# First maxima by transfers on ACT's queue, dense filler products among the first tiles, first weight slices prepared further ahead

## What is computed

```python
# attention, for each batch and head, t = 0..767
m_new  = maximum(f_gate[t] + m, i_gate[t])
f_stab = exp(f_gate[t] + m - m_new);  i_stab = exp(i_gate[t] - m_new)
C = f_stab * C + i_stab * outer(v[t], k[t])
n = f_stab * n + i_stab * k[t]
y[t] = sigmoid(o_gate[t]) * (C @ q[t]) / maximum(abs(n @ q[t]), 1.0)
...
# x: (3072, 320), w_in: (320, 2048), w_out: (2048, 320)
x = maximum(x @ w_in, 0) ** 2 @ w_out                      # first layer
h = x @ w_in2                                              # second layer
x = where(h > 0, h, exp(minimum(h, 0)) - 1) @ w_out2
```

## Time and profile before

| | us |
|---|---|
| median of 3 runs | 880.08 |
| lowest, highest | 879.46, 881.64 |
| the profiled execution, device time | 878.74 |
| its span, first to last instruction | 877.0 |

### The profile page before, as it was taken

The page is one execution under the profiler, slowest core; times in us unless marked ns, Lnnn a source line. Parts: engine busy times, 40 slices in busy tenths (PEclk is TensorE's granted clock), DMA queues, the critical chain, the costliest instruction groups (busy, mean ns, idle before and its releaser), DMA issues.

```text
span 877.0 us, 15290 instructions
## 1 busy us (share of the span) xinstructions
PE 858.6 (98%) x5633; PEld 838.5 (96%) x5633; DVE 514.6 (59%) x879; ACT 436.7 (50%) x955; POOL 379.0 (43%) x409
## 2 busy tenths in 40 slices
PE   9996899999999999999999999999999999999998
PEld 7876899999999999999999999999999999999998
DVE  4478888777678587775763764444444444444443
ACT  2274566465565565655734654434444443434343
POOL 2155564454444444543532754333334343433333
PEclk9997999999999999999999999999999999999999
DMA  6265443335354333453402410000000000000000
GB/s 166 82 213 178 133 104 100 99 104 135 90 162 108 101 99 100 108 135 102 130 4 96 117 50 1 16 10 13 11 2 23 1 23 1 24 1 23 1 24 24
DMA packets 21487, 63.86 MB, mean 73 GB/s; under 512 B 3012, under 2 KB 8996, under 8 KB 18852
## 3 DMA queue, kind: packets, MB, share of 16 engines
q1 hardware_dynamic: 21412, 62.88, 25.7%
HBM read 55.61 MB, written 4.03 MB: 68 GB/s over the span
## 4 chain that ended last, share of the span: by engine, by line
PE 91%; DVE 5%; DMA 1%; issue 1%; ACT 1%; POOL 1%; SPq 0%; DVEq 0%; ACTq 0%; POOLq 0%
PE hps L932 39%; PE acc L946 37%; PE att L849 4%; PE att L798 2%; PE att L841 2%; PE att L832 1%; PE att L854 1%; DMA x<-in_w_all 1%; PE acc L819 1%; DVE win L652 1%; PE hps L877 1%; PE att L855 1%; DVE win L651 1%; PE hps L798 0%; PE acc L807 0%
## 5 line engine op out<-in xcount | busy, mean ns | idle before, releaser
L932 PE MATMUL hps<-xth,win 128*128 128x384 f32 x1280 | 351.5, 340 | 2.2 <-DVE xtl L644 1.2
L946 PE MATMUL acc<-wout,ghi 128*128 128x320 f32 x1536 | 348.5, 313 | 0.0
L932 PE MATMUL hps<-xtl,win 128*128 128x384 f32 x768 | 260.2, 339 | 0.0
L946 PEld LDWEIGHTS acc<-wout,ghi 128*128 128x128 f32 x1536 | 259.0, 189 | 0.3 <-POOL glo L377 0.3
L946 PE MATMUL acc<-wout,glo 128*128 128x320 f32 x768 | 238.2, 310 | 0.0
L932 PEld LDWEIGHTS hps<-xth,win 128*128 128x128 f32 x1280 | 230.4, 189 | 3.0 <-DVE xtl L644 1.6
L377 POOL TENSOR_TENSOR glo<-hact,ghi 128x384 fp32r<-128x384 f32 x128 | 130.0, 1016 | 218.6 <-ACT ghi L544 218.6
L370 POOL TENSOR_TENSOR hact<-hact 128x384 f32<-128x384 f32 x128 | 109.5, 855 | 182.1 <-ACT hact L499 180.1
L748 DVE TENSOR_TENSOR glo<-hact,ghi 128x384 fp32r<-128x384 f32 x128 | 81.3, 635 | 116.1 <-POOL hact L370 115.8
L499 ACT ACTIVATE hact<-hps 128x384 f32<-128x384 f32 x128 | 62.7, 490 | 169.9 <-PE hps L932 169.9
L932 PEld LDWEIGHTS hps<-xtl,win 128*128 128x128 f32 x768 | 145.2, 189 | 0.0
(11 more groups left out here) (151 smaller groups left out, 736.3 us busy)
## 6 DMA issues: line engine op xcount, KB each, us to landing
raw<-in_qk SPq DMA_DIRECT2D x20, 960.0 KB, 7.1
kvo<-in_kvo SPq DMA_DIRECT2D x23, 484.0 KB, 7.8
wts<-m_rows SPq DMA_DIRECT2D x21, 512.0 KB, 4.8
x<-in_w_all SPq DMA_DIRECT2D x16, 352.0 KB, 6.4
wts<-in_w_all SPq DMA_DIRECT2D x12, 352.0 KB, 3.0
out_x<-hsum SPq DMA_DIRECT2D x16, 160.0 KB, 1.9
state_rows<-state SPq DMA_DIRECT2D x40, 52.5 KB
kvo<-in_w_all SPq DMA_DIRECT2D x4, 352.0 KB, 4.4
```

The lines of the kernel that those rows point to most:

```text
L932: last = nc.tensor.matmul(hps[t % 2][:, 0:NT], win[:, j, w, :], x[:, kk, :], start=(i == 0), stop=(i == len(parts) - 1))
L946: last = nc.tensor.matmul(acc[u][:, 0:DM], g[t % GR][:, cols], wout[:, j, w, :], start=(j == 0 and i == 0), stop=(j == NF - 1 and i == 2))
```

## The change

1. **First maxima.** `spread_m` for tiles 1 and 2, `pick_m` and its ones are gone. ACT writes the rows of the first chunk to DRAM (in the place of SP) and starts two transfers of 512 KB, `first_m(1)` and `first_m(2)`, that bring them back broadcast.
2. **Fillers.** 8, 5, 2, 6, 6, 2, 6, 4, 6, 6, 10 and 6 between the pieces of tiles 0 to 2, 67 in place of 13.
3. **Weights.** `EARLY` = 6: slices 0 to 5 are loaded and split ahead of step 0, slice t + 6 in step t. The remainders of w_in for slices 0 to 5 are made by POOL (a new `split_lo` there), not DVE; POOL's now count two for each slice.
4. **Tiles.** Tiles 3, 4, 5 start at steps 1, 6, 10. The last weight column of tiles 0 to 2 is copied by POOL (`keep_last`), the copy of `a_col` moves to ACT, tile 2 has its own buffers for gate and values, `out_gate(3)` moves into the loop, and the transposes of tiles 0 to 2 use bank A0.

The core of the diff; banks, semaphore lists and buffers are left out.

```diff
+EARLY = 6
...
 def start_of(g):
-    return NF * (g // T - 1) + 5 * (g % T) - (g >= 2 * T)
+    if g < 2 * T:
+        return (1, 6, 10)[g - T]
+    return NF * (g // T - 1) + 5 * (g % T) - 1
...
             load_kvo(1)
-            wait(sp, "m_ready", 1)
-            sp.dma_start(m_dram[0], ends[0:R, 3, :]).then_inc(s["m_stored"], 16)
             load_qk(2)
+            load_kvo(2)
             for n in range(RING):
                 load_w(n)
-            load_kvo(2)
             load_qk(3)
             load_m(3)
+            load_w(RING)
             wait(sp, "m_all_ready", 2)
...
+            load_w(RING + 1)
             load_kvo(3)
             load_qk(4)
             load_m(4)
+            for n in range(EARLY, RING + EARLY):
+                load_w(n)
...
+            def keep_last(g):
+                pool.wait_ge(s["masked"], g + 1)
+                nc.gpsimd.tensor_copy(last[:, g, :].unsqueeze(2), wts[g % 3][:, :, P - 1:P]).then_inc(s["last_ready"], 1)
+
+            def split_lo(n):
+                slot = raw_w(n)[0]
+                pool.wait_ge(s["win_hi"], n + 1)
+                whole = slot[:, 0:2 * P].rearrange("p (k n) -> p k n", n=P)
+                nc.gpsimd.tensor_tensor(win[:, n, 3:5, :], whole, f32(win[:, n, 0:2, :]), ALU.subtract).then_inc(s["win_lo"], 1)
+                pool.wait_ge(s["win_lo"], 2 * n + 1)
+                nc.gpsimd.tensor_tensor(win[REM:P, n, 2, :], slot[REM:P, 2 * P:3 * P], f32(win[REM:P, n, 2, :]), ALU.subtract)\
+                    .then_inc(s["win_lo"], 1)
+                pool.wait_ge(s["win_lo"], 2 * n + 2)
...
-            pick_m(1)
-            pick_m(2)
             mask(0)
+            keep_last(0)
             make_wv(0)
             mask(1)
+            keep_last(1)
+            mask(2)
+            keep_last(2)
+            split_lo(0)
             split_out_lo(0)
-            mask(2)
             make_wv(1)
+            split_lo(1)
             split_out_lo(1)
             make_wv(2)
+            split_lo(2)
             split_out_lo(2)
-            split_out_lo(3)
             mask(3)
+            for n in range(RING - 1, EARLY):
+                split_lo(n)
+                split_out_lo(n)
             make_wv(3)
...
+            def first_m(g):
+                src = m_dram[0, heads_of(g), :].rearrange("r t -> (r t)").unsqueeze(0).broadcast_to([P, HT])
+                act.wait_ge(s["m_stored"], 16)
+                act.dma_start(wts[g].rearrange("p h t -> p (h t)"), src).then_inc(m_in[g], 16)
...
+            act.wait_ge(s["m_ready"], 1)
+            act.dma_start(m_dram[0], ends[0:R, 3, :]).then_inc(s["m_stored"], 16)
+            out_gate(0)
             exponents(0, 0)
-            out_gate(0)
+            first_m(1)
             exponents(0, 1)
+            first_m(2)
+            out_gate(1)
             exponents(1, 0)
             exponents(1, 1)
-            out_gate(1)
+            out_gate(2)
             exponents(2, 0)
             exponents(2, 1)
+            act.wait_ge(s["a_ps"], 2)
+            nc.scalar.activation(a_col[:, 1:CH - 1, :].rearrange("p c r -> p (c r)"), A2[:, 0:P], ACT.Copy).then_inc(s["a_col_ready"], 1)
...
             exponents(3, 0)
             exponents(3, 1)
+            for n in range(RING, EARLY):
+                split_hi(n)
+                split_out_hi(n)
...
-                        if t + RING < NF:
-                            split_lo(t + RING)
+                        if t + EARLY < NF:
+                            split_lo(t + EARLY)
```

More of the change, by code:

```diff
@@ L89, in mlstm_two_dense_layers @@
         hsum = [sb(f"hsum_{i}", [P, H, E]) for i in range(2)]
-        gate = [sb(f"gate_{i}", [P, H, D]) for i in range(2)]
+        gate = [sb(f"gate_{i}", [P, H, D]) for i in range(3)]
         den = sb("den", [P, H])
@@ L135, in mlstm_two_dense_layers @@
         m_in = [s[f"m_in_{i}"] for i in range(3)]
-        kvo_in = [s[f"kvo_in_{i}"] for i in range(2)]
+        kvo_in = [s[f"kvo_in_{i}"] for i in range(3)]
         w_in = [s[f"w_in_{i}"] for i in range(SPARE)]
@@ L164, in score_banks, with m_loaded, gate_of @@
         def score_banks(g):
-            return {1: (hps[0], hps[1]), 2: (A0, acc[0])}.get(g, (A0, A1))
-        def m_banks(g):
-            return ((acc[0], acc[1]), (acc[2], A2), (acc[0], acc[1]))[g]
+            return {1: (hps[0], hps[1]), 2: (acc[0], acc[1])}.get(g, (A0, A1))
         def x_bank(g):
-            return acc[2] if g < T else A2
+            return A0 if g < T else A2
+        def m_loaded(eng, g):
+            eng.wait_ge(m_in[g % 3], 16 * (g // 3 + (g % 3 > 0)))
+        def gate_of(g):
+            return gate[2 if g == 2 else g % 2]
         def raw_of(g):
@@ L220, in load_kvo @@
             def load_kvo(g):
[L221 to L224, removed]
+                if g != 2:
+                    wait(sp, "intra_ps", g - 1)
+                    wait(sp, "dc_ps", to_state(max(0, g - 1)))
+                    wait(sp, "egate_ready", g - 1)
+                sp.dma_start(kvo_of(g), kvo[g]).then_inc(kvo_in[2 if g == 2 else g % 2], 16)
             def load_state(g):
@@ L236, in load_w @@
                 before = n - RING if n < NF else n - SPARE if n >= NF + SPARE else -1
-                wait(sp, "win_lo", before + 1)
+                wait(sp, "win_lo", 2 * (before + 1))
                 wait(sp, "wout_lo", before + 1)
@@ L313, in make_wv @@
                     pool.wait_ge(s["last_ready"], g + 1)
[L314 removed]
+                    column = last[:, g, :].unsqueeze(2)
                 else:
@@ L361, in _ @@
                         g = tile_at(t, -2)
-                        if g is not None and B <= g < TILES - B:
+                        if g is not None and g < TILES - B:
                             make_wv(g)
@@ L401, in out_gate @@
                 wait(act, "x_ready", g - 1)
-                nc.scalar.activation(gate[g % 2][:], o_of(g), ACT.Exp, scale=-1.0).then_inc(s["egate_ready"], 1)
+                nc.scalar.activation(gate_of(g)[:], o_of(g), ACT.Exp, scale=-1.0).then_inc(s["egate_ready"], 1)
             def exponents(g, u):
@@ L521, in _ @@
                         g = tile_at(t, -1)
-                        if g is not None and g >= B:
-                            split_state_hi(g)
+                        if g is not None:
+                            if g >= B:
+                                split_state_hi(g)
                             out_gate(g)
@@ L682, in _ @@
             weigh(1)
+            finish(0)
             dve.wait_ge(s["last_ps"], 1)
@@ L694, in _ @@
             nc.vector.tensor_copy(m0_line[:, 2:CH], m0_by_chunk[:, 1:CH - 1]).then_inc(s["m0_row_ready"], 1)
-            finish(0)
             weigh(2)
+            x_lo(0, 0, 0, A0)
+            gate_plus(2)
+            gate_recip(2)
+            finish(1)
             dve.wait_ge(s["m0_ps"], 1)
@@ L903, in _ @@
             done.then_inc(s["last_ps"], 1)
-            scores(2)
-            x1_transposed(0)
+            state_added(0)
+            keep_warm(6)
+            within(2)
             pe.wait_ge(s["m0_row_ready"], 1)
```

177 lines of the change are left out of this document (76 added, 101 removed).

## The result

| | before | after |
|---|---|---|
| median, 9 runs each | 880.08 us | 884.53 us |
| lowest, highest | 877.46, 882.67 | 883.40, 889.64 |
| ratio after / before | | 1.0071 (95%: 1.0053 to 1.0089) |
| the profiled execution, device time | 878.74 | 888.73 |
| its span | 877.0 | 887.0 |

The change made the kernel 0.7% slower, where 0.7% faster was forecast. After's nine times stand in two groups, five from 883.4 to 884.5 and four from 887.9 to 889.6; the profiled one is of the upper group. So its trace tells 10 us, of which 4 to 5 are not in every execution.

A forecast was written before the change was run, and what follows sets the result against it. It took TensorE, busy in 98% of the span, as the bound, with DVE's and POOL's chain setting its waits. 7.2 + 0.7 - 2 (clock loss) = 5.9 us off 878.74 gave 872.8, forecast as a median of 874, range 867 to 888.

The forecast's parts named there:

- What bounds the kernel: TensorE busy in 98%; it waits 6.7, 3.5, 0.7 us before transposes of tiles 3, 4, 5; nothing to win from 121 us.
- the assumption under the forecast: Tiles 0 and 1 on TensorE: fillers bring 2.4 GHz by about 6 us and hold it; fillers then take 175 ns.
- The rival with 0.14: TensorE's clock rises, falls again at about 10 us; fillers cost 320 ns; time 887 us; chance 0.14.
- (a): Up to the weights of tile 1: maxima land at 14.6 us, tile 1 weighed at 19.6, against 22.8 before.
- (b): From tile 1's weighing to tile 2's transposes: 7.3 and 9.5 us, ending at 36.4 against 49.6; gain 13.2 us.
- (c): From tile 2's transposes to the first `glo`: 13.1 us against 7.2, with 5.7 for POOL's three slices; some 6 us lost.
- (d): The steps: even up to tile 3 and for tile 4; the 0.7 us wait before tile 5's transposes goes.

The follow-up runs named there:

- long_after_b: The changed kernel with 18 fillers in place of 5 in the second group, all later fillers as in the changed kernel; one execution, 891.36 us.
- nofill: The changed kernel without the 54 later fillers, those behind the first two groups; 880.30 us, ratio 1.0004 to the kernel before.
- kvo4: The changed kernel with SP's loads for tile 4 placed ahead of those of weight slices 7 to 9; 884.81 us, ratio 1.0038.
- Poolfirst: The changed kernel with slices 3 to 5 split ahead of tile 3's mask and exponents, slice 5 loaded earlier; 882.41 us, ratio 1.0053.
- early4: The changed kernel without the 54 later fillers and with four weight slices ahead of step 0 in place of six; 878.57 us, ratio 0.9988.
- transonly: The kernel before with the store and transfers of the first maxima, spread products and picks for tiles 1 and 2 out; 875.22 us, ratio 0.9944.
- long_dense_b: The changed kernel with 18 fillers in the second group, 8 between all pieces, 4 within the spread and each tile's scores; one execution, 887.13 us.
- dense: The changed kernel with 8 fillers between pieces in place of 2 to 6, and 4 within the first spread and each tile's scores; 883.98 us, ratio 1.0057.
- all3: The changed kernel without the 54 later fillers, slices 3 to 5 ahead of tile 3's mask, tile 4's loads ahead of slices 7 to 9; 875.11 us.
- all3s: The same three edits as all3, with tiles 3, 4 and 5 at steps 0, 5 and 10 as in the kernel before; 875.37 us, ratio 0.9945.

## Why the prediction was wrong

**What bounds the kernel.** Right: all of the difference lies ahead of step 16, and the chain runs over the chunk maxima, tile 2, POOL's first square and DVE's row.

**The failing step: the assumption under the forecast.** "I assume here that fillers bring the upper level by about 6 us and hold it over tiles 0 and 1." They brought it at about 6.7 and lost it at 10.2; from there to 37.5 us TensorE was busy at 1.2 GHz and the fillers cost 320 ns each. Taking them out gives back 0.67%. The rival with 0.14 came true, at its place and nearly at its price: it put tile 2's transposes at 49.5 (51.3 measured), the first `glo` at 64 to 64.5 (65.2) and the time at 887 (884.5 median, 888.7 profiled). Its reasons stood in the rows: no fp32 work had raised the level in 44 us, and over the first spread and scores only two fillers stand. They should have weighed more than the lack of a row with a fall under work. The one trace of the kernel before could not show such a fall in this stretch, as its level was not up ahead of 54 us. Of the two things that the rival named, two fillers over the first spread and scores and groups of six later, it was behind the two that the level fell, in after and in long_after_b; the six are not tested by it.

**(a) Mis-sized, and it alone would have sunk most of the gain.** The maxima landed at 18.4, not 14.6. The store was 6.7 us against the 4 or so that (a) left it, near the 8.1 of the earlier trace rows, which I had set aside for being on another queue; the broadcast took 7.2, not 5.9. In every trace with these transfers, with fillers or without, at either level, `weigh` of tile 1 starts between 22.0 and 22.9. So tile 1 is set by the transfers, and the gain of a held level was at most what followed it. By my own sum that is 23.7 + 16.8 = 40.5 for tile 2's transposes in place of 36.4; nofill, at the low level all along, had 44.9. That left some 4 us for 54 fillers to win. Kvo4's trace comes nearest to the assumption, with the level up over the scores of tiles 0 and 1: tile 1 is weighed at 23.9 and tile 2's transposes end at 46.0, not 36.4, and that execution took 877.7.

**(b)** The length from tile 1 to tile 2's transposes was 27.6 us in after, 16.8 forecast (of whose terms the first sum is 7.2, not 7.3). The order of its parts was as told, the wait of `out_gate(2)` for `finish(0)` with it; but TensorE at the low level took the place of DVE as the path: in after DVE stands idle for 11.2 us, up to 36.5, for the transposes of the chunk maxima. In nofill it is 20.8 us, with TensorE again the later up to the chunk maxima. "The fillers in between lie in TensorE's waits" was wrong: TensorE had 1.8 us of waits there in after.

**(c) Right.** 13.9 us measured, 13.1 forecast; a slice 2.17 us, of 1.9 taken: the subtraction of 256 columns takes 0.73 and the 64 x 128 one 0.46, where their columns suggested 0.55 and 0.28. Poolfirst and early4 showed the tail to be a loss of its own.

**(d) Half right.** "Even" holds from tile 3 to tile 5: 46.0 us before, 43.1 after with one step less, where 42.5 follows from the step and the lost wait. Up to tile 3 it was 22.9 us in place of 21. I had followed SP's transfers for tiles 0 to 3 but not the queue behind the new loads of slices 6 to 11, where tile 4's values stand. The kvo4 run showed 3.6 us. TensorE waited 3.6 us in front of tile 3's transposes, not 10 or more, after 3.5 us for tile 3's weights. And the wait of 3.5 us in front of tile 4's transposes did not stay where it was: it became one of 4.1 us in front of tile 5's scores, which at steps 1, 6 and 10 stand ahead of them.

**What the parts are worth,** by the ratios: the transfers alone -0.56%; the weights, POOL's share and the rest, unmended, +0.60% on top of that (nofill against transonly); the later fillers +0.67%. In sum 0.71%, the result, as it must be, since the three lead from before to after one by one; each is uncertain by some 0.3%. The gain I had seen in the spread products was real and was spent twice over.

## What to carry to other kernels

Fillers pay only if they hold the level over the work between them and if that work is the path; measure both, in more than one execution, before adding them, since at the low level each costs 320 ns in place of 175. Work that is "prepared ahead" has to stand, on each engine, where that engine idles, and not behind the last wait ahead of the loop; and the early loads for it must not stand in a queue ahead of a transfer that is needed sooner. A transfer measured alone says little of one that is issued while 4 MB are on their way, on whatever queue.

## What the hardware did that I had not expected

- The level of TensorE fell with the engine busy throughout: 27.5 of 27.5 us busy at granted 0.50 from 10 to 37.5 us, and no wait ahead of the fall either. Two fillers (0.6 us) between the spread and the scores of tile 0 did not hold it, and groups of two to six among the fp32 work did not bring it back for 27 us. Eight fillers between all pieces and four within did hold it in long_dense_b, to 39.4 us, but not past 10.0 in dense. The Trainium skill ("TensorE: Matmul & The Clock Gate", Why this matters for your kernels) advises against idle gaps between bursts; here there was none ahead of the fall.
- Whether it rises and how long it holds differs between executions of one program: to 10.2 us in after's trace and to 18.7 in kvo4's, with the same instructions up to there. The times go with it. Of kvo4's ten, four with a mean granted clock of 0.974 to 0.979 took 877.1 to 880.2 us, two with 0.969 and 0.973 took 884.5 and 885.1, four with 0.988 or 0.990 took 886.3 to 890.2. The kernel before has two such kinds too, closer together: of its 22 executions that stand beside transonly, all3, all3s and early4, eleven with 0.963 to 0.965 took 877.6 to 879.8 us and eleven with 0.990 to 0.994 took 878.5 to 882.7. Its one trace, on which the prediction rests, is of the second kind.
- A store of 16 KB, the only transfer on ACT's queue at that time, took 6.7 us while SP's loads ran; in the kernel before one of the same size takes 1.5 us between 40 and 43 us, with little else under way (both rows below, after's first). The Trainium skill ("DMA: Bandwidth & Descriptors", Queues, rings and completion order) has the DMA engines take turns between queues; whether they did cannot be read here, but the turn, if it was taken, did not bring the store near 1.5 us.

```profile
m_rows<-x ACTq DMA_DIRECT2D x1, 16.0 KB, 6.7
m_rows<-x SPq DMA_DIRECT2D x1, 16.0 KB, 1.5
```

- DVE's split of 256 columns took 3.54 us at 81.30 in after, beside POOL's two subtractions for q, against 0.41 when POOL idles.
